# Ten more products on constants on TensorE, ahead of the first expert item

## What is computed

```python
# q, k, v: (2, 8, 768, 64); centroids: (8, 16, 64)
mask = argmax(q_n . c_n) == argmax(k_n . c_n)          # same nearest centroid
attn = softmax(where(mask, q @ k.T / 8, -1e9)) @ v
x = attn.transpose(0, 2, 1, 3).reshape(1536, 512)
logits = x @ w_gate                                    # 8 experts
e_idx = argmax(logits); gate_w = softmax(logits)[e_idx]
eom = sigmoid(x @ w_output_gate)
for e in range(8):
    m = e_idx == e
    out[m] = gate_w[m] * eom[m, e] * (relu(x[m] @ w1[e]) @ w2[e])   # 512 -> 1024 -> 512
h = out @ w_in                                         # 512 -> 2048
g = where(h >= 1, h, where(h <= -1, 0, (h + 1)**2 / 4))
result = g @ w_out                                     # 2048 -> 512
```

## Time and profile before

| | us |
|---|---|
| median of three runs | 832.93 |
| lowest and highest run | 832.7, 833.83 |
| the profiled execution | 836.38 |
| its span | 834.6 |
| TensorE busy in the span | 804.2 |
| mean granted TensorE clock | 0.984 of full |

### The profile page before, as it was taken

How to read it: one execution, slowest core, us unless ns; L and a number is a source line. 1 busy time by engine, 2 the same in 40 slices (tenths; PEclk the granted TensorE clock), 3 DMA queues, 4 the chain that set the end, 5 groups by cost and what they waited for, 6 DMA issues and landing times.

```text
span 834.6 us, 13743 instructions
## 1 busy us (share of the span) xinstructions
PE 804.2 (96%) x4370; PEld 681.0 (82%) x4371; DVE 450.1 (54%) x795; ACT 383.4 (46%) x757; POOL 347.0 (42%) x343
## 2 busy tenths in 40 slices
PE   7999999999999948999999999999999999999995
PEld 4899999999999836888888888888888888888884
DVE  5688888888888875212212212335445444555452
ACT  3788888888888845222223223212223322332222
POOL 6436654354642118678857857766000100010001
PEclk9999999999999977999999999999999999999999
DMA  4344433324111147699859859665000100010001
GB/s 108 99 118 155 121 97 101 116 66 128 48 49 35 57 131 241 217 373 327 293 201 335 269 201 349 256 227 177 1 1 1 50 1 1 0 51 1 1 0 51
DMA packets 45428, 105.43 MB, mean 126 GB/s; under 512 B 5200, under 2 KB 12880, under 8 KB 44368
## 3 DMA queue, kind: packets, MB, share of 16 engines
q1 hardware_dynamic: 29584, 60.92, 22.1%
q0 software_dynamic: 15808, 44.04, 15.8%
HBM read 92.37 MB, written 6.29 MB: 118 GB/s over the span
## 4 chain that ended last, share of the span: by engine, by line
PE 93%; ACT 3%; DVE 2%; DMA 1%; issue 1%; POOL 0%; POOLq 0%; SPq 0%; DVEq 0%
PE ps L1468 16%; PE ps L1511 15%; PE ps L1435 13%; PE ps L1455 13%; PE ps L1256 7%; PE ps L1272 4%; PE ps L1242 4%; PE ps L1243 4%; PE ps L1270 4%; PE ps L1284 3%; PE ps L1196 2%; PE ps L1445 2%; PE ps L1216 2%; PE ps L1207 1%; PE ps L1177 1%; PE ps L1413 1%
## 5 line engine op out<-in xcount | busy, mean ns | idle before, releaser
L396 POOL TENSOR_TENSOR weights<-raw_w,weights 128x2048 fp32r<-128x2048 f32 x34 | 157.2, 4627 | 47.7 <-DMA weights<-in_moe_w 35.6
L1511 PE MATMUL ps<-weights,g_t 128*128 128x512 f32 x576 | 140.8, 394 | 0.8 <-DVE g_t L1122 0.8
L1468 PE MATMUL ps<-y_t,weights 128*128 128x512 f32 x576 | 139.6, 391 | 0.0
L1511 PEld LDWEIGHTS ps<-weights,g_t 128*128 128x128 f32 x576 | 107.3, 188 | 25.1 <-DVE g_t L1122 2.1
L1468 PEld LDWEIGHTS ps<-y_t,weights 128*128 128x128 f32 x576 | 108.1, 188 | 24.0 <-POOL weights L396 0.2
L1435 PE MATMUL ps<-weights,x_t 128*128 x456 | 112.2, 402 | 1.7 <-DVE x_t L1088 1.7
L927 DVE TENSOR_TENSOR p_t<-ps,p_t 128x384 fp32r<-128x384 f32 x192 | 98.9, 551 | 27.5 <-ACT p_t L629 27.1
L567 POOL DMA_INDIRECT out<-y_sb,order_u x12 | 11.8, 982 | 236.9 <-ACT y_sb L778 235.1
L1455 PE MATMUL ps<-weights,h_t 128*128 x456 | 109.4, 395 | 0.3 <-DVE h_t L1094 0.3
L1435 PEld LDWEIGHTS ps<-weights,x_t 128*128 128x128 f32 x456 | 85.9, 192 | 20.2 <-issue 2.3
L762 ACT ACTIVATE ps<-g_a,half 128x512 f32<-128x512 f32 x48 | 33.2, 692 | 145.9 <-DVE g_b L1117 145.9
(11 more groups left out here) (178 smaller groups left out, 1080.4 us busy)
## 6 DMA issues: line engine op xcount, KB each, us to landing
raw_w<-in_moe_w SPq DMA_DIRECT2D x32, 1024.0 KB, 6.4
weights<-in_moe_w POOLq DMA_DIRECT2D x28, 1024.0 KB, 9.2
qk_t<-qk_t SPq DMA_DIRECT2D x32, 192.0 KB, 2.6
raw_w<-in_moe_w_in SPq DMA_DIRECT2D x4, 1024.0 KB, 6.1
weights<-in_moe_w_in POOLq DMA_DIRECT2D x4, 1024.0 KB, 7.8
raw_w<-in_moe_w_out SPq DMA_DIRECT2D x4, 1024.0 KB, 7.4
weights<-in_moe_w_out POOLq DMA_DIRECT2D x4, 1024.0 KB, 11.7
raw<-in_q SPq DMA_DIRECT2D x16, 192.0 KB, 2.8
```

The lines of the kernel that those rows point to most:

```text
L396: pool.tensor_tensor(weights[:, unit % 2, 1, c * CHUNK:(c + 1) * CHUNK], low_chunk(unit, c), high_chunk(unit, c).bitcast(F32), ALU.subtrac ...
L1468: last = mm(ps[:, UP_BANKS[n % 2], :], wi[:, a, k, f * P:(f + 1) * P], y_ts[g % 2][:, b, k, :], start=(k == 0 and j == 0), stop=(k == KC - ...
L1511: last = mm(ps[:, t, :], g_t[:, n % 2, a, t * P:(t + 1) * P], wo[:, b, f, :], start=(f == 0 and j == 0), stop=(f == FC2 - 1 and j == 2))
```

## The change

A fourth group of ten warm products is put into TensorE's stream, behind the wait for the tables and ahead of `item_xt(0)`. Nothing else differs; the lines behind the insertion move down by one.

```diff
@@ -72,7 +72,7 @@
 ZEROS = NT // 2
 IDLE_BANK = 3
-WARM = (11, 11, 9)
+WARM = (11, 11, 9, 10)
@@ -1484,6 +1484,7 @@
                     up(0, 0)
                 output(i, u, unit_base(i, 1), isinstance(i, int) and i < 2)
 
+            warm(WARM[3])
             item_xt(0, 0, 0, True)
             hidden(0, 0, True)
             field_rows()
```

## The result

The changed kernel takes 838.51 us in the median of 14 executions, against 833.62 for the kernel before, also over 14: the ratio is 1.0055, with a 95% interval of 1.0045 to 1.0065. Thirteen executions of the new one lie between 835.4 and 840.53, those of the old one between 832.47 and 834.3. (The fourteenth of the new kernel took 2388.85 us, and nothing explains it. It is counted among the 14 of the median, which is 838.35 without it; the ratio leaves it out.) The forecast of no change was wrong: the ten products cost 4.7 to 4.9 us, 0.6%.

The account below looks back on a forecast made before the run. TensorE, busy 96% of the span, was taken as the bound, with `output(0)` held at 334.06 by the raw weight chunk. TensorE's saving becomes waiting: +0.0 us on the 832.93 median gives 832.9, range 831.3 to 834.6.

Parts of the forecast that it names:

- Steps 1 and 2: Warm products behind the table wait: start at 311.68, ten take 2.2 to 4.25 us, until 315.93 at the low clock.
- Step 3: First transposes wait behind the warm products; hidden products start 318.76 at the latest, costing 1.1 to 2.0 us on TensorE's path.
- Step 4: Clock rise among warm products and transposes: between 315.2 and 317.8, taken at about 316.5; 0.7 of that span reached.
- Step 5: Pause of 1.7 us behind the transposes: clock falls again in early hidden products, chance two thirds; a 3.4 us stretch costs 1.7.
- Step 6: Hidden products to `output(0)`: 13.86 us, TensorE ready at 332.36 or 334.06; start stays at 334.06, sum +0.0 us.
- The bound from the weights: Before `output(0)`: expert 1's fourth raw chunk lands at 329.60; its rounding and two copies allow the start only at 334.06.
- The faster rival: Fourth raw chunk lands 1.75 us or more earlier and the clock holds, so TensorE's gain shows: 831.4 to 830.9; chance 0.18.
- The prize of about 3 us: Item 0's hidden products, 316.77 to 322.9: low clock covers 6.1 us of work that would take 3.05; 0.37% of total.
- The slower one: Transposes held up and clock not high in hidden products: +0.3 to +1.6 us, say 834.4, up to 835.4; chance 0.22.
- does not do what it says: Products on constants bring no rise, clock stays 1.2 GHz until 322.9: +0.7 us, 833.7; chance within a shared 0.22.

Follow-up runs that it names:

- a_again: The changed kernel, unaltered, run and profiled again: 838.01 us, ratio 1.0052 to the kernel before.
- e_wait1: Kernel before, no added products; TensorE also waits for the second gather before transposing the first rows: 834.96 us, ratio 1.0017.
- e_fill: Changed kernel plus five warm products behind the first transposes, filling the pause before the hidden products: 838.81 us, ratio 1.0049 to the kernel before.
- x_keep: Changed kernel plus ten warm products behind the field rows, in the new wait for ScalarE: 836.44 us, ratio 1.0034 to the kernel before.
- x_actpad: Changed kernel plus 24 small ScalarE copies ahead of the rounding of chunk 0: 837.86 us, ratio 1.004 to the kernel before.
- x_crowd: Changed kernel with raw weight chunks 2 and 3 issued only after all twelve gathers landed: 847.79 us, ratio 1.0157 to the kernel before.
- after, second: Second profile of the changed kernel, unaltered, near its median: span 837.0 us; that run's median 838.62 us, ratio 1.0055.
- before, second: Second profile of the kernel before, unaltered: span 832.0 us; that run's median 833.71 us, ratio 0.9998.
- x_hold: Changed kernel with its ten products replaced by twelve ahead of the table wait and seven behind the first transposes: 834.15 us, ratio 0.9999 to the kernel before.
- x_best: Changed kernel, warm products instead twelve ahead of the table wait and seven behind the first transposes, gathers held at the seventh: 831.52 us, ratio 0.9967.
- x_pause9: Changed kernel with the last three gathers held until item 0's first hidden half and item 1's transposes are done: 833.49 us, ratio 0.9999.
- e_early: Changed kernel with the ten products moved ahead of the wait for the tables: 833.59 us, ratio 0.9997 to the kernel before.

## Why the prediction was wrong

**Steps 1 and 2, right.** The ten products start on the table cast's signal and take 4.45 us against 4.25 forecast, at the low clock's spacing to the end, in the first and second profiles of after; in a_again they take 4.21, as the clock rises among them.

**Step 3, right.** The transposes on `xs` follow at once, and the hidden products begin 1.9 us later relative to the tables than before: the forecast had up to 2.0. In e_wait1 a delay of 1.2 us, without work, costs 1.2 us.

**Step 4, right.** The rise came 5.1 us after the products began, in the first profile of after: between 314 and 315, as these windows of 1 us show.

```profile
314.00:315.00 1.00, 0.93 (x5) 0.62 0.89 279
315.00:316.00 1.00, 0.00 (x0) 1.00 1.03 354
...
324.00:325.00 1.00, 0.00 (x0) 1.00 1.04 391
325.00:326.00 1.00, 0.00 (x0) 1.00 0.99 363
```

A mean of 0.62 puts it at 314.76. That is 0.6 us after the end of the last warm product and within the four transposes. The Trainium skill says, in "TensorE: Matmul & The Clock Gate", section "Part 4: PE-mode transpose", that transposes don't count as TensorE's work in the same way. These windows neither contradict nor prove it: the rise could be the ten products' alone. In five other profiles (a_again, e_fill, x_keep, x_actpad, x_crowd) it is: the ten take 3.75 to 4.21 us and the transposes behind them 0.60, so the clock was back before the transposes began. Whether transposes would have kept up what the products began was not tried.

**Step 5, half wrong.** The clock did not fall in the pause of 1.75 us: it was 1.00 at 315 and stayed so through the first half of `hidden(0)`. That it falls "again in the early hidden products, with chance two thirds", is refuted in all three profiles. It held in the first profile even through 3.49 us without work, and fell in the second after 2.0 of 3.42. The fall that was expected came in that one, but 9 us later and in a wait that the prediction didn't have; by the mean clocks, most executions have more low clock than the mild ones, and where is not on record.

**Step 6, the step that failed.** The sum took, from the chain of before, "the wait for the ReLU 0.67" and no more, and with it that ScalarE and VectorE see a signal of TensorE at once, at whatever moment it comes. The wait now ahead of L1445 measured 2.39, 3.49 and 3.42 us in the three profiles. In after, second, TensorE's path by the sum would have reached `output(0)` at 317.08 + 13.86 = 330.94; it did at 336.35, 5.4 later. Up to L1445 the sum has 2.89 + 0.44 + 2.81 + 0.67 = 6.81 us and the trace 9.95 (317.08 to 327.03), 3.1 more, which is the late signal. From there it has 0.87 + 5.74 + 0.44 = 7.05 and the trace 9.32, 2.3 more, which is the low clock. The two are the whole of it.

The bound from the weights, from which the forecast of zero came, was real but had little slack on the loss side. In before, second, h_t is last as in the earlier trace rows, by 0.37 us, though counted from the tables it comes 1.1 us earlier than in the first profile of before (309.85 to 331.36 is 21.5, 311.43 to 334.06 is 22.6). In after, second, VectorE had completed h_t at 331.9, and TensorE came 4.4 us later. On the gain side the bound did what the prediction said: x_hold, with TensorE 1.3 us ahead of it, waits for h_t and gains nothing that is measured. The faster rival, that the chunk may land earlier, is right for x_best alone. Its ground, that the median lies 3.45 us under the profiled time and so "something is shorter" without the profiler, does not hold: before, second, is profiled too and took 833.85, 0.14 above the median of its eight. What was long was the execution of the first profile, with its tables 1.6 us later and a low clock from 22.5 to 25.9 us, where before, second, has 1.00.

The prize of about 3 us was too large for a common execution as well: in before, second, the first half of `hidden(0)` takes 4.63 us and not 5.48.

**The rivals.** The slower one had the right sign and place (an `item_xt` that comes late, a clock that is low in the expert products) but the wrong mechanism: the clock was high in `hidden(0)`. Its highest price was 835.4; the measured median is 3.1 above that. The one that "does not do what it says" is refuted by the 3.04 us of the first half. None of the rivals had a signal that is late, so none could give the size.

**What stays open.** What holds the signals of TensorE when GpSimd's last gathers go on beside them isn't known, and neither is the part of VectorE's L1080 in it. The number of instructions, the two instruction transfers at that place, the address steps and the raw chunks are each excluded as the sole cause. Whether the profiler's own recording has a part in it is open too: the record has a span and a granted clock for every execution, so no time in it is known to be free of recording. The execution of 2388.85 us is unexplained.

## What to carry to other kernels

When a step is made faster, ask not only who waits for it but what other thing will be under way at the new moment of its signals; here the twelve hidden products, 1.6 to 2.5 us faster, moved signals of TensorE to a moment at which, with GpSimd's last gathers under way, they came late, and lost more than they had gained. A profile explains the median only if its execution is like the median: look at the time and the mean clock of every execution before reading one trace. A sum made of waits from one trace carries the chance of that trace with it: a step that is late by 3 us for a reason outside the sum is not absorbed by 0.3 us of slack. Warm products cost nothing where they end before the data comes, and here they gained (x_best, 0.33% faster) only together with late gathers held back until the signals were through.

## What the hardware showed beyond that

- A signal from TensorE left ScalarE idle for 1.5 to 3.0 us in nine profiles, where it takes about 0.03 elsewhere (319.72 to 319.75 in x_pause9); the trace gives such a wait the releaser "remote". ScalarE and VectorE are both hit: in after, second, VectorE's L1073 has "remote" too, and in e_early VectorE is idle for 3.15 us ahead of it.
- The issue of an indirect gather on GpSimd takes 0.95 us, but 2.0 to 3.0 us when VectorE's L1080 (a subtraction on 128x2048 values, 2.29 us) ends in the midst of it: 26 issues in 19 profiles, and each ends 0.8 us behind that L1080.
- The granted clock held through 1.75 and once 3.49 us without work, and in another execution of the same kernel it fell after 2.0 us of a pause of 3.42. The mean clock of an execution tells the two kinds apart: 0.989 or 0.990 goes with 834.9 to 836.2 us, 0.984 to 0.988 with 837.6 to 840.5.
